# Fifteen block products for eighteen in the first product of the second mixture-of-experts layer

## The chip, the cores and the metric

The kernel runs on one core of a Trainium2 chip. The metric is the device time of one execution in microseconds, and a verdict compares medians of timed executions.

## The reference

Attention with a decaying state gives x (3072 tokens by 384), a first layer without a router turns it into a new x, and the second layer, which the change is about, mixes eight experts:

```python
logits = x @ w_gate                       # 3072 x 8
P = np.exp(logits - logits.max())
for _ in range(8):                        # alternate row and column normalisation
    P /= P.sum(1, keepdims=True) + 1e-09
    P /= P.sum(0, keepdims=True) + 1e-09
    P *= N / E
for e in range(E):                        # E = 8, w1: 384 x 1024, w2: 1024 x 384
    h = np.maximum(x @ w1[e], 0.0)
    out += P[:, e:e + 1] * (h @ w2[e])
```

## The kernel before

All matrix products of the layers are made in a split form: a float32 number is kept as a high part (`_hi`, type fp32r) and the rest (`_lo`), and a product is three matmuls, hi by hi, hi by lo and lo by hi (`split_product`, lines 843 to 846).

The program has two stretches. In the first one (lines 1011 to 1037) attention and the first layer are interleaved in slices; at its end x lies transposed in SBUF as `x2` (3 blocks of 128 features by 3072 tokens). The second layer then runs as 48 units: expert e (8) outside, 512 tokens t (6) inside. A unit has eight steps f, one for each 128 hidden features:

- TensorE, `hidden` (L1047): 3 feature blocks by 3 matmuls of 512 columns into one of the two PSUM banks of `psH`;
- ScalarE (L563): relu of that bank into `h_hi`; VectorE (L791): the rest into `h_lo`;
- TensorE, `project` (L1060), one step behind: 4 token blocks j by 3 matmuls of 384 columns. Here the tokens are the stationary operand, so that y comes out with tokens on the partitions, in the four banks of `psY`, where it stays through the unit.

After a unit VectorE multiplies each `psY` bank with that token's share `Pm` and adds it to `acc` (L821). The weights of an expert come in one DMA of 3 MB, `wx_raw`; ScalarE and VectorE split them for the next expert between their other work (`split_weights`). The normalisation of P (`over_rows`, `over_columns`, eight times) lies on VectorE in the first two units, one iteration a step, with one small matmul each time (`add_columns`, L1044). GpSimd does four casts and the maximum over partitions (L397) and nothing after. The output goes out by four DMAs of 192 KB at the end (L338), the rest before.

The order on each engine is the order of the code; between engines there are only semaphores. Units after the opening are hardware loops (`Fori`).

## Time and profile before

| | us |
|---|---|
| median of 3 runs (2159.74 to 2161.33) | 2160.88 |
| the profiled execution's own time | 2158.51 |
| its span, first to last instruction | 2156.7 |
| TensorE (PE) busy | 2129.9 |
| VectorE (DVE) busy | 772.6 |
| ScalarE (ACT) busy | 572.2 |
| GpSimd (POOL) busy | 83.3 |

The granted TensorE clock is 1.000 over the whole span. A matmul's duration in a row contains its way through the array, so consecutive matmuls overlap; their pace is the distance between the starts. The same holds, less strongly, for the other engines.

### The profile page before, as it was taken

What the parts mean: (1) busy time and instruction counts of PE and PEld (TensorE: products, weight loads), DVE (VectorE), ACT (ScalarE), POOL (GpSimd) and SP (SyncE); (2) the same over time, 40 slices, a digit from 0 to 9 for tenths busy, and PEclk for the clock granted to TensorE, in tenths of its full rate; (3) what the DMA queues carried; (4) which work ended last, traced back from release to release, by engine and by line L of the source; (5) the groups of instructions that cost most, each with busy time, mean ns of one, the idle gap of its engine ahead of it and who ended that gap; (6) DMA issues with size and microseconds to landing.
All of it is one profiled execution on the core that took longest, in us unless ns stands there. A gap on an engine that the chain in (4) does not pass through costs nothing.

```text
span 2156.7 us, 41592 instructions
## 1 busy us (share of the span) xinstructions
PE 2129.9 (99%) x17692; PEld 1934.5 (90%) x17692; DVE 772.6 (36%) x1321; ACT 572.2 (27%) x1032; POOL 83.3 (4%) x99
## 2 busy tenths in 40 slices
PE   7899999999999999999999999999999999999999
PEld 4699999999899999999999999999999999999998
DVE  3666666663632322232223222222322232223222
ACT  4555556553311211121112112111211121112111
POOL 2111121111000000000000000000000000000000
PEclk9999999999999999999999999999999999999999
DMA  8411212101100010010001000100000010000000
GB/s 201 82 43 33 56 43 51 47 5 62 60 1 0 0 59 0 0 58 0 0 0 58 0 0 0 58 0 0 29 30 0 0 58 0 0 0 15 15 29 29
DMA packets 28919, 60.53 MB, mean 28 GB/s; under 512 B 3728, under 2 KB 26000, under 8 KB 27792
## 3 DMA queue, kind: packets, MB, share of 16 engines
q1 hardware_dynamic: 28128, 58.52, 9.4%
q8 instruction: 83, 1.36, 0.3%
q10 hardware_dynamic: 688, 0.48, 0.1%
q14 instruction: 20, 0.16, 0.0%
HBM read 53.09 MB, written 4.72 MB: 27 GB/s over the span
## 4 chain that ended last, share of the span: by engine, by line
PE 98%; DMA 1%; DVE 0%; issue 0%; SPq 0%; ACT 0%; DVEq 0%
PE ps L844 30%; PE ps L846 30%; PE ps L845 30%; PE ps L917 2%; PE ps L867 2%; PE ps L956 1%; PE ps L958 1%; DMA w_raw<-moe_w 1%; PE ps L939 1%; PE ps L928 0%; PE ps L879 0%; PE ps L911 0%; PE ps L856 0%; DMA R<-rT 0%; PE ps L1001 0%
## 5 line engine op out<-in xcount | busy, mean ns | idle before, releaser
L791 DVE SCALAR_TENSOR_TENSOR h_lo<-ps,h_hi 128x512 fp32r<-128x512 f32 x384 | 265.7, 692 | 1076.9 <-ACT h_hi L563 1076.5
L563 ACT ACTIVATE h_hi<-ps 128x512 fp32r<-128x512 f32 x384 | 230.3, 600 | 1317.8 <-PE ps L846 1317.8
L846 PE MATMUL ps<-wx_hi,h_lo 128*128 128x384 f32 x1536 | 517.6, 337 | 0.0
L844 PE MATMUL ps<-wx_hi,h_hi 128*128 128x384 f32 x1536 | 516.9, 337 | 0.0
L845 PE MATMUL ps<-wx_lo,h_hi 128*128 128x384 f32 x1536 | 515.5, 336 | 0.0
L846 PE MATMUL ps<-x_hi,wx_lo 128*128 (+1 forms) x1152 | 454.9, 395 | 0.0
L845 PE MATMUL ps<-x_lo,wx_hi 128*128 (+1 forms) x1152 | 454.1, 394 | 0.0
L844 PE MATMUL ps<-x_hi,wx_hi 128*128 (+1 forms) x1152 | 448.6, 389 | 0.0
L844 PEld LDWEIGHTS ps<-wx_hi,h_hi 128*128 128x128 f32 x1536 | 288.6, 188 | 14.9 <-issue 0.2
L845 PEld LDWEIGHTS ps<-wx_lo,h_hi 128*128 128x128 f32 x1536 | 288.3, 188 | 14.4
L846 PEld LDWEIGHTS ps<-wx_hi,h_lo 128*128 128x128 f32 x1536 | 288.1, 188 | 0.0
L846 PEld LDWEIGHTS ps<-x_hi,wx_lo 128*128 128x128 f32 x1152 | 216.0, 188 | 46.1
L845 PEld LDWEIGHTS ps<-x_lo,wx_hi 128*128 128x128 f32 x1152 | 216.1, 188 | 37.6
L844 PEld LDWEIGHTS ps<-x_hi,wx_hi 128*128 128x128 f32 x1152 | 216.5, 188 | 35.8
L844 PE MATMUL ps<-x_hi,wab_hi 128*128 128x256 f32 x576 | 171.7, 298 | 0.0
L846 PE MATMUL ps<-x_hi,wab_lo 128*128 128x256 f32 x576 | 162.9, 283 | 0.0
L845 PE MATMUL ps<-x_lo,wab_hi 128*128 128x256 f32 x576 | 162.8, 283 | 0.0
L402 ACT ACTIVATE Rpad<-R 64x512 f32<-64x512 f32 (+1 forms) x170 | 110.5, 650 | 142.8 <-DVE R L640 135.7
L844 PEld LDWEIGHTS ps<-x_hi,wab_hi 128*128 128x128 f32 x576 | 109.8, 191 | 4.7 <-issue 1.9
L821 DVE SCALAR_TENSOR_TENSOR acc<-ps,Pm,acc 128x384 f32 (+1 forms) x168 | 92.8, 611 | 55.9 <-PE ps L846 55.6
L845 PEld LDWEIGHTS ps<-x_lo,wab_hi 128*128 128x128 f32 x576 | 109.9, 191 | 0.1
L846 PEld LDWEIGHTS ps<-x_hi,wab_lo 128*128 128x128 f32 x576 | 109.8, 191 | 0.0
(100 smaller groups left out, 1589.1 us busy)
## 6 DMA issues: line engine op xcount, KB each, us to landing
wx_raw<-w SPq DMA_DIRECT2D x8, 3072.0 KB, 10.2
K<-kT SPq DMA_DIRECT2D x24, 192.0 KB, 3.8
R<-rT SPq DMA_DIRECT2D x24, 192.0 KB, 4.5
V<-v_rows SPq DMA_DIRECT2D x12, 384.0 KB, 3.2
Wt<-wT SPq DMA_DIRECT2D x22, 192.0 KB, 3.9
w_raw<-moe_w SPq DMA_DIRECT2D x8, 512.0 KB, 11.3
out<-acc SPq DMA_DIRECT2D x5, 768.0 KB, 3.5
wab_raw<-moe_w SPq DMA_DIRECT2D x4, 576.0 KB, 11.7
```

Source lines behind the costliest of these rows:

```text
L402: return nc.scalar.activation(dst, src, ACT.Copy)
L563: nc.scalar.activation(h_hi[:, f % RING, :], psH(f), ACT.Relu).then_inc(h_hi_made, 1)
L791: ve.scalar_tensor_tensor(out=h_lo[:, f % RING, :], in0=psH(f), scalar=0.0, in1=h_hi[:, f % RING, :].bitcast(f32), op0=ALU.max, op1=ALU.su ...
L821: ve.scalar_tensor_tensor(out=rows, in0=psY(j), scalar=share, in1=rows, op0=ALU.mult, op1=ALU.add).then_inc(y_added, 1)
L844: mm(o, w_hi, x_hi, start=start, stop=False, skip_group_check=shared)
L845: mm(o, w_hi, x_lo, start=False, stop=False, skip_group_check=shared)
L846: return mm(o, w_lo, x_hi, start=False, stop=stop, skip_group_check=shared)
L867: last = mm(ps[:, W_bank(f), 0:D], w3T[m // HB % TURNED][:, j % HB, :], wout_raw[:, j, :], start=(j == 0), stop=(j == NF - 1))
L917: last = mm(o, keys, r, start=True, stop=True)
L939: last = mm(ps[rows:rows + HROW, tail_bank(c), HD * g:HD * g + HD], Ktok[:, c, P * g + rows:P * g + rows + HROW], V[u % 2][:, c, head:head ...
L956: last = mm(o[h], V[u % 2][:, c, head:head + HD], AT[:, 2 * (NCH * g + c) + h, :], start=True, stop=(before is None))
L958: last = mm(o[h], before[:, g, :], Rpad[u % 2][:, g, h, CH * c:CH * c + CH], start=False, stop=True)
```

## The change

**The products.** For a group of three hidden blocks f and 1024 tokens (two halves of 512), the before kernel makes 3 x 3 x 2 = 18 block products of 128 x 128 weights with 128 x 512 tokens. The new one makes 15, `S1, R1, S2, R2, S3, R3, S4, R4, S5, Q1, S6, Q0, S7, Q5, S8`, numbered 0 to 14 in the order in which TensorE makes them. Each multiplies a sum of weight blocks with a sum of x blocks. The sums of x (`xs_hi`, `xs_lo`, 15 tiles of 512 tokens) are made once for each stretch of 1024 tokens, three times in all; the sums of weights (8 of 128 columns, and 7 single blocks) for each group. The 64 blocks f of the eight experts (NF2) are run as one series: one block alone by six products (`multiply_first`), then 21 groups. So there are 3 stretches of 22 groups G, 63 of them full.

**The banks.** Only two PSUM banks serve the products: even numbers S (bank 0), odd numbers R (bank 1). Some products start a bank anew and others add to what stands in it. Product p waits until p - 2 has been taken out of its bank; S1 follows S8 in the same bank. Six products are copied out by ScalarE (`COPIED`), nine are added to or subtracted from tiles `tb` in SBUF by VectorE (`ADDED`). From the ninth product on each step finishes one of the six hidden tiles b (`LAST_ADDED`); ScalarE then makes `h_hi` and VectorE, one step later, `h_lo`, now both from SBUF.

**The second product** is turned: w2 is stationary and 512 tokens of h are moving, y comes out transposed in six banks, one for each half T and feature block d, and stays there through all eight blocks f of an expert. A projection (3 matmuls) follows each product, two of them after S3, Q1 and S8, 14 projections behind at the start of a group. When an expert ends, VectorE multiplies each of the six banks with `Pb`, P spread over the partitions, into a ring `tmp` of four (`take_y`), and GpSimd adds that to `acc`, which takes the place of x2 (`add_y`). Since eight is no multiple of three, the six `take_y` fall in three places: at R4 to Q0 of a group (6 experts), at S7 to R1 of the next (9), at S2 to S4 (8), and at the very end (1).

**GpSimd** now makes the sums of x and of weights and all low parts of the w1 operands, adds y, and has the maximum over partitions between. P goes through DRAM once and comes back broadcast, 512 KB for each expert and stretch. The rows of `acc` are turned back on TensorE: 48 transposes of 128 columns beside the next stretches, 24 at the end. The loops are written out, nothing is a hardware loop. The sums of P over rows stay where TensorE needs them in bank 1, so each of the eight column sums holds an R product back until `cs_taken`.

```diff
-    RING = 2
-    PU = NF - 1 + NJ
+    NF2 = E * NF
+    NG = 1 + (NF2 - 1) // 3
+    SINKHORN = 8
+    S1, R1, S2, R2, S3, R3, S4, R4, S5, Q1, S6, Q0, S7, Q5, S8 = range(15)
+    X_OWN = {S1: 1, R3: 2, S5: 5}
+    X_SUM = {R1: (0, 1), R2: (2, 1), R4: (2, 3), Q1: (1, 3), S6: (5, 2), Q0: (0, 2), S7: (4, 5), Q5: (3, 5), S8: (2, 4)}
+    X_LESS = (R2, S6)
+    ADDED = {S3: 1, R4: 2, S5: 4, Q1: 0, S6: 2, Q0: 1, S7: 3, Q5: 4, S8: 5}
+    LAST_ADDED = {Q1: 0, S6: 2, Q0: 1, S7: 3, Q5: 4, S8: 5}
+    FINISHED = [0, 2, 1, 3, 4, 5]
+    W2_RING, TMP = 4, 4
...
+            upto = lambda q: q + 1 + (q >= S3) + (q >= Q1)
+            if G % NG == 0:
+                return max(0, 3 * block_no(G) - upto(Q0) + p + 1)
+            return max(0, 3 * block_no(G) - upto(Q0) + upto(p) + (p == S8))
+        COLUMNS_AT = [(1, S6), (1, S8), (2, S1), (2, S6), (2, S8), (3, S1), (3, S6), (3, S8)]
...
+            def add_y(n):
+                T, d = y_tile(n)
+                pool.wait_ge(y_taken, n + 1)
+                if n // 6 % E == 0:
+                    pool.wait_ge(p_loaded, 16 * (n // 6 + 1))
+                    gp.tensor_tensor(y_acc(n), y_acc(n), Pb[:, T, :], ALU.mult).then_inc(y_added, 1)
+                else:
+                    pool.wait_ge(y_added, n - 5)
+                    plus(y_acc(n), y_acc(n), tmp[:, tmp_no(n) % TMP, :]).then_inc(y_added, 1)
+                    continue
+                if G > 1:
+                    sum_late(G)
+                    split_late(G)
+                ys = [n for p in range(NP) for n in ys_after((G, p))]
+                soon = [n for n in ys if y_at[n][1] <= S3 and n >= 6]
+                for n in soon:
+                    add_y(n)
+                if g == NG - 1 and st + 1 < NST:
+                    sum_first(st + 1)
+                    sum_xw(st + 1)
+                    for p in x_summed_in(st + 1):
+                        sum_x(st + 1, p)
+                    split_first(st + 1)
+                if full_no(G) + 1 < (NG - 1) * NST:
+                    after = full_at(full_no(G) + 1)
+                    sum_early(after)
+                    split_early(after)
+                for n in ys:
+                    if n >= 6 and n not in soon:
+                        add_y(n)
...
-                    u = e * NT + t
-                    act.wait_ge(hidden_made, u * NF + f + 1)
-                    if not (opening and f < RING):
-                        act.wait_ge(proj_done, proj_after(u, f - RING) if f >= RING else proj_after(u - 1, f - RING + NF))
-                    nc.scalar.activation(h_hi[:, f % RING, :], psH(f), ACT.Relu).then_inc(h_hi_made, 1)
...
+
+            def take_h(G, p):
+                b = LAST_ADDED[p]
+                act.wait_ge(added, add_no(G, p))
+                free_slot(G, b)
+                nc.scalar.activation(h_hi[:, b, :], tb[:, t_of(G, b), :], ACT.Relu).then_inc(h_hi_made, 1)
+                for p in range(NP):
+                    if p in COPIED:
+                        copy_product(G, p)
+                    if p in LAST_ADDED:
+                        take_h(G, p)
+                    if p == R2 and G > 1:
+                        take_late(G)
+                    if G == 1 and p == R2:
+                        route()
+                    if (G, p) == P_TURN:
+                        act.wait_ge(p_turned_made, 1)
+                        copy(p_turned[0:NTT // 2 * E, :, :], ps[0:NTT // 2 * E, 1, 0:2 * P].rearrange("p (h t) -> p h t", t=P)).then_inc(p_copied, 1)
+                    if p == S4:
+                        take_w2(G)
+                    if p == S6 and g + 1 < NG:
+                        take_early(full_at(full_no(G) + 1))
+                    if g == NG - 1 and st + 1 < NST:
+                        if p == S3:
+                            take_first(st + 1)
+                        if p >= 2:
+                            take_xs(st + 1, p - 2)
...
-                for f in range(NF):
-                    dve.wait_ge(h_hi_made, u * NF + f + 1)
-                    ve.scalar_tensor_tensor(out=h_lo[:, f % RING, :], in0=psH(f), scalar=0.0, in1=h_hi[:, f % RING, :].bitcast(f32),
-                                            op0=ALU.max, op1=ALU.subtract).then_inc(h_split, 1)
-                        ve.scalar_tensor_tensor(out=rows, in0=psY(j), scalar=share, in1=rows, op0=ALU.mult, op1=ALU.add).then_inc(y_added, 1)
...
+            def add_product(G, p):
+                b = ADDED[p]
+                t, bank = tb[:, t_of(G, b), :], bank_of(p)
+                dve.wait_ge(multiplied, product_no(G, p))
+                if p in (S3, R4, S7, S8):
+                    ve.tensor_tensor(t, t, bank, ALU.subtract).then_inc(added, 1)
+            def split_h(G, b, what):
+                dve.wait_ge(h_hi_made, h_no(G, b))
+                ve.scalar_tensor_tensor(out=h_lo[:, b, :], in0=what, scalar=0.0, in1=h_hi[:, b, :].bitcast(f32),
+                                        op0=ALU.max, op1=ALU.subtract).then_inc(h_split, 1)
+            def take_y(n):
+                T, d = y_tile(n)
+                dve.wait_ge(projected, last_projection(n) + 1)
+                    dve.wait_ge(p_loaded, 16 * (n // 6 + 1))
+                    if m >= TMP:
+                        dve.wait_ge(y_added, y_of_tmp(m - TMP) + 1)
+                    ve.tensor_tensor(tmp[:, m % TMP, :], ps[:, y_bank(T, d), :], Pb[:, T, :], ALU.mult).then_inc(y_taken, 1)
...
+                for p in range(NP if g else NL1):
+                    if step_before.get((G, p)) in COLUMNS_AT:
+                        over_columns(it)
+                    if g and p in ADDED:
+                        add_product(G, p)
+                    if split_now is not None:
+                        split_h(G, split_now, tb[:, t_of(G, split_now), :])
+                        split_now = None
+                    if g and p in LAST_ADDED:
+                        split_now = LAST_ADDED[p]
+                    for n in ys_after(step_before.get((G, p))) if (G, p) in step_before else ():
+                        take_y(n)
+                    if g and p == Q1:
+                        split_w2(G)
+                    if g == NG - 1 and st + 1 < NST and p >= 3:
+                        split_xs(st + 1, p - 3)
...
-                for k in range(KD):
-                    cols = slice(P * k, P * k + P)
-                    last = split_product(psH(f), wx_hi[:, f, cols], wx_lo[:, f, cols], high[:, k, :], x2_lo[:, k, x], k == 0, k == KD - 1)
-                last.then_inc(hidden_made, 1)
-                    last = split_product(psY(j), h_hi[:, f % RING, toks], h_lo[:, f % RING, toks],
-                                         wx_hi[:, f, D:2 * D], wx_lo[:, f, D:2 * D], f == 0, f == NF - 1)
...
+                if p >= S2:
+                    if p - 2 in COPIED:
+                        pe.wait_ge(copied, copy_no(G, p - 2))
+                    else:
+                        pe.wait_ge(added, add_no(G, p - 2))
+                elif G % NG == 1:
+                    pe.wait_ge(h_split, h_no(G - 1, p))
+                else:
+                    pe.wait_ge(added, add_no(G - 1, S8 if p == S1 else Q5))
+                triple(bank_of(p), w_hi, w_lo, xs_hi[:, p, :], xs_lo[:, p, :], p in (S1, R1, Q1, Q0, Q5), True).then_inc(multiplied, 1)
...
+                if d == 0:
+                    pe.wait_ge(w2_split, m + 1)
+                    pe.wait_ge(h_split, h_no(G, b))
+                if f % NF == 0:
+                    y = 6 * (E * (G // NG) + f // NF - 1) + 3 * (1 - T) + d
+                    if y >= 0:
+                        pe.wait_ge(y_taken, y + 1)
...
+                for p in range(NP):
+                    multiply(G, p)
+                    if (G, p) in COLUMNS_AT:
+                        add_columns(COLUMNS_AT.index((G, p)))
+                    if (G, p) == P_TURN:
+                        turn_p()
+                    project_to(projections(G, p))
+                if G in PUT_AT:
+                    done_st, j = PUT_AT[G]
+                    pe.wait_ge(y_added, 6 * E * (done_st + 1))
+                    pe.wait_ge(added, add_no(G, Q5))
+                    turn_rows(j, 1)
...
```

On TensorE, in the middle of a unit, the last matmuls of `hidden` and the first of `project` before:

```order
L846 MATMUL ps<-x_hi,wx_lo 128x512
L844 MATMUL ps<-x_hi,wx_hi 128x512
L845 MATMUL ps<-x_lo,wx_hi 128x512
L846 MATMUL ps<-x_hi,wx_lo 128x512
L1062 REGISTER_ALU
L844 MATMUL ps<-wx_hi,h_hi 128x384
L845 MATMUL ps<-wx_lo,h_hi 128x384
L846 MATMUL ps<-wx_hi,h_lo 128x384
L844 MATMUL ps<-wx_hi,h_hi 128x384
L845 MATMUL ps<-wx_lo,h_hi 128x384
```

and in a full group now, where L1438 to L1440 are the three matmuls of `triple` (`xs` a product, `h` a projection, `own` and `sum` the weight operands of w1, `w_hi` here the tile of w2):

```order
L1440 MATMUL ps<-xs_hi,sum_lo 128x512
L1438 MATMUL ps<-h_hi,w_hi 128x512
L1439 MATMUL ps<-h_lo,w_hi 128x512
L1440 MATMUL ps<-h_hi,w_lo 128x512
L1438 MATMUL ps<-xs_hi,own_hi 128x512
L1439 MATMUL ps<-xs_lo,own_hi 128x512
L1440 MATMUL ps<-xs_hi,own_lo 128x512
L1438 MATMUL ps<-h_hi,w_hi 128x512
L1439 MATMUL ps<-h_lo,w_hi 128x512
L1440 MATMUL ps<-h_hi,w_lo 128x512
L1438 MATMUL ps<-xs_hi,own_hi 128x512
L1439 MATMUL ps<-xs_lo,own_hi 128x512
```

Nine and twelve matmuls between changes of work have become three and three, all of 512 columns, and each product begins with a wait for a bank.

On VectorE, in the first unit of an expert before (L607 are the low parts of the next weights, L791 `split_h`, L821 the four additions of y):

```order
L791 SCALAR_TENSOR_TENSOR h_lo<-ps,h_hi 128x512
L607 TENSOR_TENSOR wx_lo<-wx_raw,wx_hi 128x768
L791 SCALAR_TENSOR_TENSOR h_lo<-ps,h_hi 128x512
L607 TENSOR_TENSOR wx_lo<-wx_raw,wx_hi 128x768
L791 SCALAR_TENSOR_TENSOR h_lo<-ps,h_hi 128x512 x6
L821 SCALAR_TENSOR_TENSOR acc<-ps,Pm,acc 128x384 x4
```

and in group 6 now, from product S5 to S7, where an expert ends (L1173 and L1169 `add_product`, L1177 `split_h`, L996 the low parts of w2, L1190 `take_y`):

```order
L1171 TENSOR_TENSOR tb<-ps,tb 128x512
L1190 TENSOR_TENSOR tmp<-ps,Pb 128x512
L1173 TENSOR_TENSOR tb<-ps,tb 128x512
L1190 TENSOR_TENSOR tmp<-ps,Pb 128x512
L996 TENSOR_TENSOR w_lo<-w_raw,w_hi 128x384 x3
L1173 TENSOR_TENSOR tb<-ps,tb 128x512
L1177 SCALAR_TENSOR_TENSOR h_lo<-tb,h_hi 128x512
L1190 TENSOR_TENSOR tmp<-ps,Pb 128x512 x2
L1173 TENSOR_TENSOR tb<-ps,tb 128x512
L1177 SCALAR_TENSOR_TENSOR h_lo<-tb,h_hi 128x512
L1190 TENSOR_TENSOR tmp<-ps,Pb 128x512
L1169 TENSOR_TENSOR tb<-tb,ps 128x512
```

The six `take_y`, which stood together after a unit, now stand between the additions that free the product banks; the fifth and sixth wait for GpSimd's first and second `add_y`, because `tmp` has four places.

On GpSimd, at the start of the second layer before:

```order
L389 MEMSET wg 128x96
L390 MEMSET ones 128x128
L393 CAST wx_hi<-wx_raw 128x768
L395 CAST x_hi<-x_49 128x1536
L393 CAST wx_hi<-wx_raw 128x768
L395 CAST x_hi<-x_49 128x1536
L397 ISA
L397 ISA allmax<-rowmax 128x1
```

and now, in the last group of the first stretch (G = 21): `split_late`, then the sums for the next 1024 tokens (`first_sum`, `xw`, `xs_sum`):

```order
L578 TENSOR_TENSOR own_lo<-w_raw_125,own_hi 128x128
L578 TENSOR_TENSOR own_lo<-w_raw_125,own_hi 128x2x128
L578 TENSOR_TENSOR sum_lo<-w_sum,sum_hi 128x512
L578 TENSOR_TENSOR first_sum<-first_raw 128x128 x2
L578 TENSOR_TENSOR first_sum<-first_sum,first_raw 128x128
L581 TENSOR_TENSOR xw<-x_49 128x512
L581 TENSOR_TENSOR xw<-xw,x_49 128x512
L581 TENSOR_TENSOR xs_sum<-x_49 128x512
L581 TENSOR_TENSOR xs_sum<-xw,x_49 128x512
L578 TENSOR_TENSOR xs_sum<-x_49 128x512
```

GpSimd was empty from there on; now 38 instructions and more stand in such a group. ScalarE in the same group (L834 `take_xs`, the high parts of the new x sums; L717 copies) has the first of the sums between the late weights and the copy of product R3:

```order
L717 ACTIVATE own_hi<-w_raw_125 128x128
L717 ACTIVATE own_hi<-w_raw_125 128x2x128
L717 ACTIVATE sum_hi<-w_sum 128x512
L834 ACTIVATE xs_hi<-xs_sum 128x512
L717 ACTIVATE first_hi<-first_raw 128x384
L717 ACTIVATE first_hi<-first_sum 128x256
L834 ACTIVATE xs_hi<-xs_sum 128x512
L717 ACTIVATE tb<-ps 128x512
```

The copy of R3 (the last row) stands behind the waits of `take_xs` and `take_first` for GpSimd's sums.

## Rows read from the trace of the kernel before

**Rows 1.** The page: the chain that ended last, by engine and by line.
```profile
PE 98%; DMA 1%; DVE 0%; issue 0%; SPq 0%; ACT 0%; DVEq 0%
PE ps L844 30%; PE ps L846 30%; PE ps L845 30%; PE ps L917 2%; PE ps L867 2%; PE ps L956 1%; PE ps L958 1%; DMA w_raw<-moe_w 1%; PE ps L939 1%; PE ps L928 0%; PE ps L879 0%; PE ps L911 0%; PE ps L856 0%; DMA R<-rT 0%; PE ps L1001 0%
```
**Rows 2.** PE's waits between 480 and 640 us: total, times, longest.
```profile
PE ps L1044 <- DVE csum L773: 0.6, 1, 0.6
```
**Rows 3.** Stretches: length, then busy us (instructions) by engine; PEclk, DMA share, GB/s.
```profile
0.00:400.00 400.00, 377.05 (x7349) 338.56 (x7350) 242.82 (x466) 218.39 (x422) 68.04 (x79) 1.00 0.31 71
1000.00:1500.00 500.00, 500.00 (x2515) 453.77 (x2514) 131.49 (x196) 83.71 (x136) 0.00 (x0) 1.00 0.03 13
```
**Rows 4.** PE in order of time: start, duration, line; hidden and projection of one step.
```profile
621.86 0.39 PE L844 MATMUL ps<-x_hi,wx_hi 128*128 x1
...
623.71 0.39 PE L846 MATMUL ps<-x_hi,wx_lo 128*128 x1
623.94 0.33 PE L844 MATMUL ps<-wx_hi,h_hi 128*128 128x384 f32 x1
...
626.04 0.39 PE L844 MATMUL ps<-x_hi,wx_hi 128*128 x1
```
**Rows 5.** Groups by line: count | busy, mean ns | idle before, releaser.
```profile
L791 DVE SCALAR_TENSOR_TENSOR h_lo<-ps,h_hi 128x512 fp32r<-128x512 f32 x384 | 265.7, 692 | 1076.9 <-ACT h_hi L563 1076.5
L563 ACT ACTIVATE h_hi<-ps 128x512 fp32r<-128x512 f32 x384 | 230.3, 600 | 1317.8 <-PE ps L846 1317.8
L607 DVE TENSOR_TENSOR x_lo<-x,x_hi 128x512 fp32r<-128x512 f32 x3 | 2.0, 685 | 0.0
L393 POOL CAST wx_hi<-wx_raw 128x768 fp32r<-128x768 f32 x2 | 1.7, 828 | 8.0 <-DMA wx_raw<-w 8.0
L395 POOL CAST x_hi<-x 128x1536 fp32r<-128x1536 f32 x2 | 3.1, 1568 | 0.0
```
**Rows 6.** ACT, POOL and DVE in order of time, around 563, 162 and 195 us.
```profile
562.80 0.60 ACT L563 ACTIVATE h_hi<-ps 128x512 fp32r<-128x512 f32 x1 [2.31 <-PE ps L846]
563.29 0.84 ACT L402 ACTIVATE wx_hi<-wx_raw 128x768 fp32r<-128x768 f32 x1
...
162.29 1.26 POOL L376 CAST x_hi<-xT 128x768 fp32r<-128x768 f32 x1 [4.36 <-DMA xT<-yT]
...
162.17 0.69 DVE L640 TENSOR_TENSOR R<-R,decay 128x512 f32<-128x512 f32 x1
162.77 1.32 DVE L642 TENSOR_TENSOR K<-K,decay 128x512 f32<-128x512 f32 x1
...
194.08 2.13 POOL L359 COPY Rpad<-R 64x1024 f32<-64x1024 f32 x2 [26.11 <-PE ps L958]
...
195.24 1.25 DVE L607 TENSOR_TENSOR ab_lo<-ab,ab_hi 128x256 fp32r<-128x256 f32 x1 [3.21 <-ACT ab_hi L402]
```
**Rows 7.** Opening of the second layer: PE, DVE, POOL, ACT in order of time.
```profile
543.67 0.40 PE L844 MATMUL ps<-x_hi,wx_hi 128*128 128x512 f32 x1
...
552.29 0.36 DVE L799 TENSOR_REDUCE rowmax<-ps 128x1 f32<-128x192 f32 x1 [0.39 <-PE ps L1008]
...
552.75 0.36 POOL L397 PARTITION_ALL_REDUCE allmax<-rowmax  x1 [33.14 <-DVE rowmax L799]
...
559.11 0.19 ACT L566 ACTIVATE negmax<-allmax 128x1 f32<-128x1 f32 x1
```
**Rows 8.** DVE in order of time: one normalisation of P.
```profile
569.21 0.17 DVE L778 TENSOR_SCALAR cden<-ps 128x8 f32<-128x8 f32 x1
...
571.37 0.55 DVE L773 TENSOR_REDUCE csum<-Pm 128x8 f32<-128x192 f32 x1
```
**Rows 9.** PE in order of time: four transposes of 128 columns.
```profile
26.50 0.66 PE L856 MATMUL ps<-const_sb,w_raw 128*128 128x128 f32 x4 [0.29 <-DMA w_raw<-moe_w]
```
**Rows 10.** The end: last matmul, and the last output DMAs with median time to landing.
```profile
2153.08 0.34 PE L846 MATMUL ps<-wx_hi,h_lo 128*128 128x384 f32 x1
...
2152.78 1.92 SPq L338 DMA_DIRECT2D out<-acc  x4
```

796 lines of the change are left out of this document (547 added, 249 removed).

## The prediction, made before the changed kernel was run

> **What bounds the kernel now.** I read the chain that ended last first [rows 1]: 98% of it is TensorE, and its three long lines are the split matmuls. The list of PE's waits comes next [rows 2]: in 160 us around the start of the second layer there is one wait, 0.6 us, and from 640 us on the list is empty. The stretches say the same: 500.00 us of 500 busy with 2515 matmuls, VectorE and ScalarE at 131 and 84 us, GpSimd at nothing [rows 3]. So the second layer is a pure stream of matmuls, and its time is their number times their pace. The clock is granted at its upper level, 2.4 GHz, throughout.
>
> The pace is the distance between starts [rows 4]. Nine matmuls of 512 columns take 623.94 - 621.86 = 2.08 us, 0.2311 us each; the twelve of 384 columns after them take 626.04 - 623.94 = 2.10 us, 0.175 each. A unit has 72 and 96 of them: 16.6 + 16.8 = 33.4 us, and 500 us / 2515 x 168 gives 33.4 too. 48 units are 1603 us.
>
> **What the change removes on TensorE.** Products: 3 x (6 + 21 x 15) = 963 triples. Projections: 3 x 64 x 6 = 1152 triples. Together 6345 matmuls of 512 columns, at 0.2311 us 1466 us. That is 137 us less, 121 of it from the 567 products saved, the rest since the projections go in fewer, longer matmuls. The pace of a 512-column form is in the trace, so the bound of this term is only 3 us either way. That a wait comes every three matmuls instead of nine I cost at nothing while it is fulfilled: the last product before a change, which carries the semaphore, is followed after 0.23 us like every other [rows 4].
> The Trainium skill, TensorE: Matmul & The Clock Gate, "The cost: per-tile semaphore tail", gives 26 ns for each increment. By that rule, with 2115 increments for about 912, the sum would be 32 us higher; the row shows no such gap, and it is a rival below.
>
> The written-out program costs nothing either: in the first 400 us, also written out, PE fetched and ran 7349 matmuls [rows 3], three times as dense as the second layer will be.
>
> **The other engines' prices.** A 512-wide VectorE operation takes 0.69 us to its end from PSUM and 0.685 from SBUF [rows 5], and the next starts 0.60 later (162.17 and 162.77 in [rows 6]); ScalarE 0.60, next after 0.50 [rows 5, 6]. From a product's last start to a reader's result I count 0.3 + 0.69 us. No GpSimd operation with two tensor inputs is in the trace. Nearest are the casts, one input: 0.83 us for 768, 1.57 for 1536 [rows 5], so 0.14 + 0.9 ns a column, 0.6 us for 512. Below it can't be; three times that, 1.8, is my upper bound. It has to read twice as much, so I take twice the column price: 1.1 us for 512, 0.83 for 384, 0.37 for 128. The Trainium skill, GPSIMD Engine Reference, "Elementwise — side-by-side cycle accounting", has 4497 ns for 2048 columns of such an add, which is an estimate of 1.1 us for 512 and would leave the sum as it is.
>
> The second price is a conflict: a VectorE operation with two SBUF inputs waits for a running GpSimd one. `ab_lo`, 256 wide, took 1.25 us beside a GpSimd copy, longer than the 0.69 of twice the width, and of two 512-wide products the one beside a GpSimd cast took 1.32 us instead of 0.69, and that cast 1.26 for 768 columns instead of 0.83 [rows 5, 6]. Before, `h_lo` was read from PSUM; now it has two SBUF inputs, six times a group.
>
> **A full group, replayed.** A step is a product and a projection, 6 x 0.2311 = 1.39 us, three steps have 2.08: 22.9 us. Count from the end of Q1. VectorE adds Q1 at 0.3, splits w2 until 2.3, adds S6 2.37, splits 2.97, adds Q0 3.76, splits 4.36 to 5.05. ScalarE is done with the next early weights at 4.8, and GpSimd's `split_early` wants 0.83 + 0.37 + 1.1 us: its first runs 5.05 to 5.88 behind that split. VectorE's next split waits until 5.88, the add of Q5 ends 7.13, the last split meets the 512-wide GpSimd one (6.9 to 8.0), and S8, ready at 7.9, is added by 9.3. S1 could start 2 projections after S8, at 9.02: **0.3 us lost a group, 19 us for 63**. If GpSimd comes a little later the order turns and nothing is lost; bounds 5 and 60. ScalarE (12 x 0.5 and some 5 us of weights) and GpSimd (about 11 us of 22.9) have room.
>
> **Ends of experts.** In the 6 groups where an expert ends at R4 to Q0, VectorE's fifth `take_y` needs GpSimd's first `add_y`, which stands behind `split_early` (done at about 8.0): 9.1. The adds of S6 and Q0 are through, but the add of S7, for which product S8 waits, stands behind that `take_y`: S8 starts 3.6 us late. The next splits run against GpSimd's adds of 1.1 and cost 1.9 more at S1: 5.5 x 6 = 33. Nine experts end at S7 to R1: one `take_y` before the add of S8, 0.8 x 9 = 7. Eight at S2 to S4, where VectorE has gaps: 2. **42 us**, bounds 15 and 85.
>
> **Opening.** GpSimd has 13 operations of 512 columns and 25 smaller ones, about 30 us, before the first group. It begins with the last eight slices, 8 x 27 matmuls of 256 columns at about 0.12 us or 26 us, and the first block adds 543.67 [rows 7] + 6 x 0.69 + 1.9 for what lies between = 549.7: just in time. In the first group the steps have no projections up to R4, 0.69 us against 0.95 for a copy: 1 us. The maximum over partitions took no longer than 559.11 - 552.65 = 6.5 us to reach ScalarE before [rows 7], and nobody waited; now ScalarE's copy of R3 is behind it, and product R4 could start at 555.6: I take 4, bounds 1 and 8. The normalisation is 2.7 us of VectorE (569.21 to 571.92 in [rows 8]): R product Q0 waits for `cs_taken` and the adds behind it are late, 2 us x 3; at S1 of groups 2 and 3 the second column sum comes only one step after the first, 3.3 x 2; turning P, 2. **19 us**, bounds 10 and 30.
>
> **The two changes of stretch.** ScalarE's copy of R3 stands behind the first x sum; GpSimd gets there after its late weights, at about 9.5 us before the end of Q1 plus 2 x 2.2 + 1.1 + 2 x 1.1 + 1.1: 5 us late. Then 10 more sums of 1.1 us and 15 VectorE splits share one port, and the first product of the new stretch waits for `split_first` behind the last sum: 6 more. **11 x 2 = 22 us**, bounds 10 and 45.
>
> **Small ones.** Transposes: (0.66 - 0.27) / 3 = 0.13 us each [rows 9], 48 are 6 us, with waits 8 (5 to 14). The tail before was 2156.7 - 2153.3, about 3.4 us, one VectorE operation and a 192 KB DMA of 1.92 us [rows 10]. Now come three more GpSimd adds that lag behind PE's pace (1.1 against 0.69), transposes and copies: **+5** (3 to 9).
>
> **The sum**, made against the profiled execution's 2158.5 (its span is 2156.7): -137 + 19 + 42 + 19 + 22 + 8 + 5 = -22, 2136.5. The median shown is 2.4 us above that execution, so I expect 2139.
>
> **The rivals.**
> 1. The forecast, stalls of 90 to 135 us: 2110 to 2156. Chance 0.41.
> 2. The work beside PE stays hidden. For it: the averages leave room everywhere (VectorE about 13 us of 22.9), the conflicts depend on who comes first, and a late stream opens slack for the next group. Against it: the in-order queue in front of S8's add has no slack in steps S6 to S8. All terms at their low bounds: 5 + 15 + 10 + 10 + 5 + 3 = 48 of 137, 2160.9 - 89 = 2072; I put this case at 2070 to 2110. Chance 0.28.
> 3. GpSimd becomes the bound: slower. If a 512-wide GpSimd operation takes 1.8 us, `split_early` needs 3.9 us instead of 2.3, is done 1.6 us later than above, just after S1's nominal start, and each VectorE split beside it waits up to 1.8: about 1.7 us lost a group instead of 0.3, +88, and the adds at expert ends, the sums between stretches grow by 0.7 x (6 x 4 + 2 x 12) = 34: 2139 + 122 = 2261. It decides from 0.3 + (22 + 4) / 63 = 0.7 us a group on. Against it: the casts' own 0.9 ns a column. Chance 0.21.
> 4. The increments show (the page's rule above): some 1200 x 26 ns, 2139 + 32 = 2171. The starts in [rows 4] speak against it. Chance 0.03.
> 5. The change doesn't do what it says, because the products' pace falls back: a matmul that waits for its bank restarts the array, say 0.3 us at each of 963 products, 289 us; [rows 2, 4] show changes of bank without a gap, so I leave it within the 0.21.
> Between 2156.5 and 2165 lies what a measurement of this kernel can't tell from no change (0.2% of 2160.9 is 4.3 us): chance 0.07.
>
> **Range.** Faster 0.41 + 0.28 = 0.69, same 0.07, slower 0.21 + 0.03 = 0.24. For 8 in 10 I leave 0.07 below 2080 and 0.13 above 2193, inside rivals 2 and 3. The forecast's own range is 2110 to 2156.
>
> **What the profile after would show.** PE's matmuls (17692 of the whole kernel before) fewer by 48 x 168 - 6345 = 1719, plus 74 transposes; 0.231 us between starts within a group; PE busy near 2000 us, and about 100 us in waits, which it hardly had: for VectorE's `tb` (L1169) at S1, the longest group; in the six groups named, waits of 2 to 4 us at S8 and a VectorE idle in front of L1190 released by POOL; some 5 us for ScalarE's `tb` in groups 21 and 43. GpSimd about 750 us busy, with 1.1 us a 512-wide `x2`. Wrong would make me: a pace other than 0.231; `h_lo` from SBUF at 0.69 without the 1.2 us ones (rival 2); GpSimd operations of 0.6 us (rival 2) or 1.8 (rival 3); waits of PE for `w1_split` rather than for `tb`.

## The result, and the profile after

The change made the kernel 1.5% slower. Median of 4 executions 2192.76 us (2190.82 to 2194.69) against 2160.31 (2159.73 to 2161.33): ratio 1.015, interval 1.0132 to 1.0167. I had put 2139 and a range of 2080 to 2193, with 0.24 for slower. That 2192.8 still lies in that range, by 0.2 us, is luck: the forecast was a gain, and its own range ended at 2156. One of the four executions of the run on the changes of stretch below fell into a slow state of the chip (3301.67 us at a granted clock of 0.557) and is left out of its numbers.

The page of after: busy times, then the chain that ended last, by engine and by line.

```profile
PE 2048.4 (93%) x16047; PEld 1688.8 (77%) x16047; DVE 1298.6 (59%) x2007; ACT 999.4 (46%) x1982; POOL 1160.8 (53%) x1553
...
PE 59%; POOL 16%; issue 12%; DVE 9%; ACT 2%; DMA 1%; POOLq 0%; ACTq 0%; DVEq 0%; SPq 0%
```

The chain was 98% TensorE before [rows 1]. Now a quarter of it is GpSimd and VectorE. The same stretch as in [rows 3]:

```profile
1000.00:1500.00 500.00, 464.99 (x1965) 370.75 (x1964) 293.30 (x405) 217.88 (x431) 329.10 (x448) 0.98 0.22 58
```

TensorE is idle for 35 of 500 us, GpSimd went from nothing to 329 us, and the clock is no longer granted in full (0.98). PE's waits in the second layer (540 us to the end), which were a single one of 0.6 us in [rows 2]: total, times, longest.

```profile
PE ps L1438 <- DVE tb L1169: 72.0, 61, 3.6
PE ps L1438 <- ACT tb L717: 15.2, 4, 6.4
PE ps L1438 <- POOL first_lo L578: 6.7, 3, 3.1
PE ps L1513 <- DVE csum L1142: 6.3, 2, 3.3
```

The account of the second layer, from the starts of its matmuls: 6345 of them, the first at 544.23, the last at 2180.7 (before: 543.67 and 2153.08). Their distance is 0.231 us (median), so 1465.7 us of the 1636.5 is the stream; 171 us is lost. Some 20 us of that is not waiting but matmuls at half the pace (below). The tail behind the last matmul is 10.2 us instead of 3.6. So 544.2 + 1465.7 + 171 + 10.2 makes the span of 2190.9.

Where the 171 us are: group lengths, from the first matmul of S1 to the next group's. A plain group (one without an expert's end, behind the opening and away from the changes of stretch) has 99 matmuls, a stream of 22.87 us.

| groups (count) | us each | lost, us | predicted |
|---|---|---|---|
| what a plain group loses, counted for groups 6 to 64 but for the four of the last line (55) | 23.25 | 21 | 19 |
| end of an expert at R4 to Q0 (6), and the groups behind | 30.4, then 23.2 or 24.6 | 47 more | 33 |
| end at S7 to R1 (8, the ninth is in the opening), and the groups behind | 23.8, then 25.5 | 22 more | 7 |
| end at S2 to S4 (8) | 25.0 | 14 more | 2 |
| groups 0 to 5, the opening | 6.2, 23.4, 32.9, 32.2, 25.1, 25.7 | 32 | 19 |
| groups 21, 22 and 43, 44, the changes of stretch | 38.3 and 10.4 | 35 | 22 |

Group 6, where the first of the six ends lies: GpSimd, VectorE and TensorE in order of time (start, duration).

```profile
709.15 1.88 POOL L578 TENSOR_TENSOR own_lo<-w_raw,own_hi 128x384 fp32r<-128x384 f32 x2 [6.24 <-ACT sum_hi L717]
...
709.58 1.12 DVE L1177 SCALAR_TENSOR_TENSOR h_lo<-tb,h_hi 128x512 fp32r<-128x512 f32 x1
...
710.99 1.26 POOL L578 TENSOR_TENSOR sum_lo<-w_sum,sum_hi 128x512 fp32r<-128x512 f32 x1
712.21 8.33 POOL L581 TENSOR_TENSOR x<-x,tmp 128x512 f32<-128x512 f32 x6
713.60 0.69 DVE L1190 TENSOR_TENSOR tmp<-ps,Pb 128x512 f32<-128x512 f32 x1 [2.90 <-POOL x L581]
714.21 0.68 DVE L1169 TENSOR_TENSOR tb<-tb,ps 128x512 f32<-128x512 f32 x1
714.80 1.69 DVE L1177 SCALAR_TENSOR_TENSOR h_lo<-tb,h_hi 128x512 fp32r<-128x512 f32 x1
...
714.94 0.50 PE L1438 MATMUL ps<-xs_hi,sum_hi 128*128 128x512 f32 x1 [3.56 <-DVE tb L1169]
```

One reads it from the bottom up. Product S8 waits 3.56 us for the add of S7 (L1169). That add could have run at 711, but in VectorE's queue the fifth `take_y` (L1190) is ahead of it. `take_y` waits 2.90 us for the first of GpSimd's six adds, which starts only at 712.21, behind `split_early` (709.15 to 712.25). The `h_lo` that follow take 1.69 us beside the adds instead of 0.69.

What happens to TensorE's clock there (length, then busy us and instructions of PE, PEld, DVE, ACT, POOL; granted clock, DMA share, GB/s):

```profile
707.00:711.00 4.00, 3.72 (x17) 2.73 (x15) 3.71 (x6) 2.40 (x5) 1.85 (x3) 1.00 0.54 154
711.00:714.70 3.70, 0.38 (x2) 0.00 (x0) 1.10 (x2) 0.00 (x0) 3.70 (x5) 1.00 0.00 0
716.30:719.70 3.40, 1.92 (x5) 0.83 (x3) 3.40 (x5) 0.63 (x1) 3.40 (x3) 0.50 0.15 39
```

TensorE stood from 711.4 to 714.9, and from 716.3 on the clock is granted at 0.50, its lower level of 1.2 GHz, when TensorE has work again. There are 14 such stretches from the opening on, 66.9 us, each behind TensorE's idle times or at the end: in groups 2 and 3, behind all six ends at R4 to Q0, at both changes of stretch. Some 100 matmuls in them started about 0.43 us apart instead of 0.231: about 10 us behind the six ends, 7 at the changes of stretch, 4 in the opening. Before, the clock was 1.00 throughout.

The prices (count | busy, mean ns | idle before):

```profile
L1177 DVE SCALAR_TENSOR_TENSOR h_lo<-tb,h_hi 128x512 fp32r<-128x512 f32 x378 | 370.3, 983 | 11.5 <-ACT h_hi L930 11.0
L581 POOL TENSOR_TENSOR x<-x,tmp 128x512 f32<-128x512 f32 x126 | 173.4, 1405 | 35.5 <-DVE tmp L1190 35.5
L578 POOL TENSOR_TENSOR sum_lo<-w_sum,sum_hi 128x512 fp32r<-128x512 f32 x126 | 162.2, 1287 | 0.0
...
L1190 DVE TENSOR_TENSOR tmp<-ps,Pb 128x512 f32<-128x512 f32 x126 | 82.7, 682 | 60.6 <-PE ps L1440 30.4 <-POOL x L581 30.2
```

Alone, GpSimd takes 1.26 to 1.31 us for 512 columns with two inputs (priced 1.1), and `h_lo` 0.98 in the mean instead of the 0.69 of [rows 5]. `tmp`, which is read from PSUM, stays at 0.68.

### The profile page after: what moved, and what is told of

Same layout as the page of the kernel before. It is cut to its first block, busy times and chain, and to the rows that moved or that the text cites. A ratio compares the mean times of both kernels' runs of the same rounds, so it can differ in the third digit from the quotient of the medians.

```text
span 2190.9 us, 41117 instructions
## 1 busy us (share of the span) xinstructions
PE 2048.4 (93%) x16047; PEld 1688.8 (77%) x16047; DVE 1298.6 (59%) x2007; ACT 999.4 (46%) x1982; POOL 1160.8 (53%) x1553
## 4 chain that ended last, share of the span: by engine, by line
PE 59%; POOL 16%; issue 12%; DVE 9%; ACT 2%; DMA 1%; POOLq 0%; ACTq 0%; DVEq 0%; SPq 0%
PE ps L1438 13%; PE ps L1440 12%; PE ps L1439 12%; PE ps L1242 5%; PE ps L1243 4%; PE ps L1244 4%; DVE h_lo L1177 4%; POOL w_sum L578 4%; POOL x L581 3%; POOL own_lo L578 3%; PE ps L1315 2%; POOL sum_lo L578 2%; PE ps L1265 2%; DVE tb L1169 2%; POOL w_sum L581 1%
## 5 line engine op out<-in xcount | busy, mean ns | idle before, releaser
L930 ACT ACTIVATE h_hi<-tb 128x512 fp32r<-128x512 f32 x378 | 236.4, 629 | 523.6 <-DVE tb L1173 373.8
L1438 PE MATMUL ps<-h_hi,w_hi 128*128 128x512 f32 x1152 | 460.0, 399 | 0.2 <-DVE h_lo L1177 0.2
L1440 PE MATMUL ps<-h_hi,w_lo 128*128 128x512 f32 x1152 | 459.8, 399 | 0.0
L1439 PE MATMUL ps<-h_lo,w_hi 128*128 128x512 f32 x1152 | 456.2, 396 | 0.0
L1169 DVE TENSOR_TENSOR tb<-tb,ps 128x512 f32<-128x512 f32 x252 | 172.1, 683 | 465.5 <-PE ps L1440 461.8
L1177 DVE SCALAR_TENSOR_TENSOR h_lo<-tb,h_hi 128x512 fp32r<-128x512 f32 x378 | 370.3, 983 | 11.5 <-ACT h_hi L930 11.0
L717 ACT ACTIVATE tb<-ps 128x512 f32<-128x512 f32 x378 | 225.1, 598 | 322.7 <-PE ps L1440 315.8
L1438 PE MATMUL ps<-xs_hi,sum_hi 128*128 128x512 f32 x504 | 207.1, 411 | 77.1 <-DVE tb L1169 72.0
L1439 PEld LDWEIGHTS ps<-h_lo,w_hi 128*128 128x128 f32 x1152 | 222.4, 193 | 49.9
L1438 PEld LDWEIGHTS ps<-h_hi,w_hi 128*128 128x128 f32 x1152 | 219.3, 190 | 52.8 <-issue 4.4
L1440 PEld LDWEIGHTS ps<-h_hi,w_lo 128*128 128x128 f32 x1152 | 219.4, 190 | 48.7
L1440 PE MATMUL ps<-xs_hi,sum_lo 128*128 128x512 f32 x504 | 201.5, 400 | 0.0
L1173 DVE TENSOR_TENSOR tb<-ps,tb 128x512 f32<-128x512 f32 x252 | 173.3, 688 | 43.9 <-PE ps L1440 40.1
L1438 PE MATMUL ps<-xs_hi,own_hi 128*128 128x512 f32 x441 | 176.9, 401 | 20.3 <-ACT tb L717 15.2
L1438 PEld LDWEIGHTS ps<-xs_hi,sum_hi 128*128 128x128 f32 x504 | 95.2, 189 | 126.6 <-issue 69.4
L1440 PE MATMUL ps<-xs_hi,own_lo 128*128 128x512 f32 x441 | 175.6, 398 | 0.0
L717 ACT ACTIVATE Rpad<-R 64x512 f32<-64x512 f32 (+1 forms) x170 | 110.5, 650 | 142.7 <-DVE R L1029 135.2
```

The lines of the kernel that those rows point to most:

```text
L717: return nc.scalar.activation(dst, src, ACT.Copy)
L930: nc.scalar.activation(h_hi[:, b, :], tb[:, t_of(G, b), :], ACT.Relu).then_inc(h_hi_made, 1)
L1169: ve.tensor_tensor(t, t, bank, ALU.subtract).then_inc(added, 1)
L1173: ve.tensor_tensor(t, bank, t, ALU.add).then_inc(added, 1)
L1177: ve.scalar_tensor_tensor(out=h_lo[:, b, :], in0=what, scalar=0.0, in1=h_hi[:, b, :].bitcast(f32), op0=ALU.max, op1=ALU.subtract).then_inc ...
L1438: mm(o, w_hi, x_hi, start=start, stop=False, skip_group_check=True)
```

## The experiments

Two theories. **Queues** (theory 1 in the expectations): what stands ahead of what on GpSimd and VectorE makes the waits, and the clock falls behind them. **Port** (theory 2): GpSimd's operations with two inputs and VectorE's from SBUF keep each other waiting, so that the work costs the same wherever it stands. All runs change only the second layer. A number of microseconds "less" is against the 2192.76 of the kernel after. The group lengths of all of them are in one table behind the last run.

### Two adds earlier

```diff
                     sum_early(after)
+                    for n in ys:
+                        if n >= 6 and y_at[n][1] in (R4, S5):
+                            soon.append(n)
+                            add_y(n)
                     split_early(after)
```

> Only GpSimd's order changes: in the six groups in which an expert ends at R4 to Q0, its first two adds of y stand ahead of split_early (where GpSimd is idle for 6 us) instead of behind it. Theory 1 (the queue in front of the add that S8 waits for is the cause of these groups' 30.4 us, and the clock's fall to 1.2 GHz follows from the idle TensorE): the wait of 3.7 us at S8 is gone, the S1 behind it is late by less than 1 us, the six stretches at the lower clock behind these groups are gone; a group takes 24 to 25 us, and the time falls by 28 to 38 us, to about 2160. Rival (the cost is GpSimd's own price and the shared port, and the work only lands elsewhere): the wait moves to S7, Q5 or the next S1 and the time falls by less than 10 us.

2171.32 us (2167.65 to 2175.29), 21 less. The six groups take 26.6 instead of 30.4 us; their waits of 3.7 at S8 are 0.7 now, and none of the clock's falls behind these groups is left. But S7 and Q5 now wait 0.5 and 0.9 us (0 and 0.4 in after): `w_lo` and `h_lo` meet the adds. TensorE's longest wait for `add_product` is 1.8 instead of 3.6 us:

```profile
PE ps L1442 <- DVE tb L1173: 49.8, 60, 1.8
```

So the queue theory holds for the long wait and for the clock, and 21 of the 28 to 38 us that I expected come; the new waits take the rest. (In the total of stretches at the lower clock the six are made up for by others, 62.0 us; two of them lie in the first layer, at 21 and 66 us, and come and go between executions.)

### All adds placed between the weights' work

```diff
+            PLACES = {R4: "ccdAAA", S7: "dAAAcc", S2: "abcccd"}
...
                     sum_late(G)
+                    adds(G, "a")
                     split_late(G)
+                adds(G, "b")
...
                     sum_early(after)
+                    adds(G, "c")
                     split_early(after)
+                adds(G, "d")
```

Capital letters, and the last two of S7, mean the next group; `tmp` has five buffers.

> All adds of y are given places between GpSimd's four weight steps, by the step at which the expert ends, with at most one behind split_early, and tmp gets a fifth buffer. Theory 1: groups with an expert's end cost 0.5 to 1 us over a plain one, so of about 50 + 22 + 14 us lost there 60 to 70 are won, with the clock: 2192.8 - 65 = about 2128, between 2120 and 2140. Rival: the adds beside VectorE's splits cost the same wherever they stand: 2155 or more.

2171.36 us (2169.66 to 2173.24): no more than the two adds alone, and the rival (2155 or more) was right, not the forecast of 2128. The groups behind S7 ends gain 0.8 us, those with S2 ends lose 1.1 (S7 waits 1.75 us where adds run beside VectorE's splits). Moved along GpSimd's queue, the adds met other operations of VectorE.

### GpSimd light

```diff
-                less(own_lo[:, 1:4, :], raw[:, 2:5, :], own_hi[:, 1:4, :].bitcast(f32))
+                gp.memset(own_lo[:, 1:4, :].bitcast(f32), 0.0)
...
-                    plus(y_acc(n), y_acc(n), tmp[:, tmp_no(n) % TMP, :]).then_inc(y_added, 1)
+                    plus(y_acc(n)[:, 0:16], y_acc(n)[:, 0:16], tmp[:, tmp_no(n) % TMP, 0:16]).then_inc(y_added, 1)
```

> GpSimd's low parts of the first product's weights become fills with zero (no input), and its adds and products for y take 16 of 512 columns; order and waits stay. Leaves out: the low parts of these weights and most of the sum over experts. Theory 2 (GpSimd's two-input operations, by their length and by holding up VectorE's splits with two SBUF inputs, make most of the lost time): h_lo takes 0.69 us beside them, the 0.4 us lost at S1 of a plain group goes, S8's wait falls under 0.5 us, and the time falls by 80 to 110 us, to 2085 to 2110; what stays is the opening and the two changes of stretch, whose sums are not touched. Rival (the order of the queues alone costs it, whatever the operations take): S8's wait stays above 2 us and the time falls by less than 40 us.

2088.22 us (2084.66 to 2089.72), 105 less, within the 80 to 110 forecast. The kernel leaves out the low parts of these weights and most of the sum over the experts. Order and semaphores are those of after, yet S8 waits 0.6 us in the six groups, plain groups lose nothing, and no fall of the clock follows them. So it is the length of GpSimd's operations, by the queue and by the port, and not the order by itself. The six groups still take 25.1 us, 2.2 more than plain ones. Three rows show length and port (the first is a wait: total, times, longest):

```profile
PE ps L1438 <- DVE tb L1169: 9.4, 17, 0.8
...
L1177 DVE SCALAR_TENSOR_TENSOR h_lo<-tb,h_hi 128x512 fp32r<-128x512 f32 x378 | 280.9, 752 | 0.2
...
L639 POOL MEMSET sum_lo<- 128x512 f32 x63 | 33.2, 527 | 0.0
```

The opening (26.8 a group) and the changes of stretch (36.7) mostly stayed, as expected.

### VectorE's splits with one input

```diff
-                ve.scalar_tensor_tensor(out=h_lo[:, b, :], in0=what, scalar=0.0, in1=h_hi[:, b, :].bitcast(f32),
-                                        op0=ALU.max, op1=ALU.subtract).then_inc(h_split, 1)
+                ve.tensor_scalar(h_lo[:, b, :], what, 0.0, 0.001, ALU.max, ALU.mult).then_inc(h_split, 1)
```

and `w2_lo` likewise. Neither is the real low part any more, but a scaled copy.

> VectorE's h_lo and w2_lo become operations with one input (max and a small factor), so that the part below the high one is not computed but a scaled copy; GpSimd is untouched at its two inputs. Theory 2a (VectorE and GpSimd wait for each other only where both read two SBUF inputs): VectorE's splits take under 0.7 us throughout, GpSimd's 512-wide adds stay near 1.27 us without the ones of 1.7, plain groups lose under 0.1 us at S1; the wait at S8 in six groups stays (it is GpSimd's queue), shorter by about 0.5 us; the time falls by 25 to 45 us, to 2150 to 2168. Rival 2b (any VectorE operation from SBUF conflicts): the splits still show 1.1 to 1.8 us and the time falls by less than 10 us.

2129.08 us (2127.09 to 2130.85), 64 less: more than either theory. VectorE in group 6 of this run, in order of time:

```profile
699.75 0.42 DVE L1177 TENSOR_SCALAR h_lo<-tb 128x512 fp32r<-128x512 f32 x1
...
701.88 1.14 DVE L1177 TENSOR_SCALAR h_lo<-tb 128x512 fp32r<-128x512 f32 x1
...
707.12 1.42 DVE L1177 TENSOR_SCALAR h_lo<-tb 128x512 fp32r<-128x512 f32 x1
```

Theory 2a has fallen: these operations have one input and still take 1.14 and 1.42 us beside GpSimd. Alone they take 0.42, not 0.69 as with two inputs; with 378 of them I take that for what was won, together with shorter holds for GpSimd's adds (1.45 beside them instead of 1.71). No run separates the two. The S8 wait stayed at 3.5 us, as the queue theory has it, and with it the clock's fall in five of the six groups.

The Trainium skill, SBUF — State Buffer, "SBUF: two separate sides", says that VectorE and GpSimd share a pair of ports as an exclusive lock held for a whole instruction, taken by a VectorE operation with two SBUF inputs or in a two-port mode; VectorE: DVE Perf Modes, "Mode 2×_2P — use both read ports for one tensor", says that this mode is one tensor read through both ports. The rows agree: 0.42 us for a lone one-input split, 1.14 and 1.42 beside GpSimd. I had used the first half of that rule and forgotten the second.

### The adds of y on VectorE, the rest as it was

```diff
+            ADDS = {S7: [(1, R1), (1, R1), (1, S2), (1, S2), (1, R2), (1, R2)],
+                    R4: [(0, S5), (1, R1), (1, R1), (1, S2), (1, S2), (1, R2)],
+                    S2: [(0, R2), (0, S3), (0, R3), (1, R1), (1, R1), (1, S2)]}
...
+                    for n in adds_at.get((G, p), ()):
+                        add_y(n)
```

This stands in VectorE's loop, with an `add_y` of its own; (1, R1) is step R1 of the next group. `tmp` has five buffers.

> The changed kernel with one thing undone in part: the adds of y (126 of 512 columns, all but those of the first and the last expert) are VectorE's again, one behind the first product of y, the others in the gaps that VectorE has at R1 to R2 and R3; tmp has five buffers. GpSimd keeps the sums and low parts of weights. Theory (GpSimd's adds, 1.27 us each in a queue with the weights and on the shared port, are what the ends of experts cost): the groups with R4 ends take 24.5 instead of 30.4 us, those behind S7 ends 23.4 instead of 25.5, S2 ends 23.5 instead of 25, plain groups stay at 23.25: about 75 us less, 2118, between 2105 and 2135. Rival (VectorE has no room for 12 operations of 0.6 us in such a group): 2160 or more.

2135.36 us (2133.99 to 2136.51), 57 less and now under the kernel before: 0.989 (0.9875 to 0.9906). The forecast was 2118, between 2105 and 2135. The groups behind S7 ends take 23.3 us and those with S2 ends 23.2: nothing of theirs is left. R4 ends are 26.3 instead of my 24.5: Q5 waits 0.9 us and S8 0.7 there with no add on GpSimd. VectorE's own queue is fuller there than I thought (GpSimd light left 25.1 us), but two `h_lo` of group 6 still met GpSimd's low parts (1.12 and 0.99 us), and the run doesn't separate the two. The list of waits, with the first row of after at 27 instead of 72 us:

```profile
PE ps L1452 <- DVE tb L1162: 26.9, 57, 1.7
PE ps L1452 <- ACT tb L710: 15.1, 4, 6.4
```

### The weights' low parts on VectorE

```diff
-                    if g and p == Q1:
+                    if g and p == R4:
                         split_w2(G)
+                    if g and p == R3 and G > 1:
+                        split_late(G)
+                    if p == Q1 and 0 < g < NG - 1:
+                        split_early(full_at(full_no(G) + 1))
```

in VectorE's loop, and GpSimd's calls gone; ScalarE takes the early weights at S5 instead of S6.

> The low parts of the first product's weights are made by VectorE (behind R3 and behind Q1 of a group, where it has room) and no longer by GpSimd, ScalarE takes the early weights at S5 instead of S6, w2 is split behind R4; GpSimd keeps the sums of weights and the adds of y, which now follow each y at once. The same work, moved away from S7 to S1 where VectorE's own splits have no slack. Theory 2 (port conflict and GpSimd's price at that place): plain groups 22.9 instead of 23.25 us, the six groups with an end at R4 to Q0 at most 26 instead of 30.4, the others 23.5; about 2192.8 - 22 - 35 - 20 = 2115, between 2105 and 2135. Rival: VectorE, with 3.3 us more a group, becomes what TensorE waits for: 2180 or more.

2147.83 us (2146.14 to 2153.98), 45 less, not the 78 of the forecast (2115, between 2105 and 2135). Plain groups are 22.9, as expected: the 0.4 us of each was `split_early` beside `h_lo`. The six are at 26.3. Two things I had not counted. S2 ends got worse, 26.5, since four adds ahead of `sum_early` now hold back the low parts in VectorE's queue; and in group 1 VectorE's wait for the weights of group 2 stands ahead of the normalisation, 7.0 us at Q0.

```profile
PE ps L1458 <- DVE sum_lo L994: 13.0, 16, 2.1
PE ps L1458 <- DVE cden L1145: 8.2, 3, 7.0
```

### The changes of stretch

```diff
                     sum_late(G)
+                    if g == NG - 1 and st + 1 < NST:
+                        for p in (R1, S2, R2):
+                            sum_x(st + 1, p)
                     split_late(G)
...
-                    sum_first(st + 1)
-                    sum_xw(st + 1)
-                    for p in x_summed_in(st + 1):
+                    for p in (S4, R4, Q1, S6, Q0, S7, Q5):
                         sum_x(st + 1, p)
-                    split_first(st + 1)
```

`sum_first`, `sum_xw` and `split_first` stand behind groups 10 and 12 of a stretch, the sum for S8 behind `sum_early`, and ScalarE takes S8's x behind the first h.

> At the two changes of stretch only: the sums of the first block and xw are made by group 10 and 12, the sums of x follow each product's end (three of them ahead of split_late, S8's behind sum_early), and ScalarE takes S8's x behind the first h. If the order of GpSimd's queue makes the 6.5 us wait at R4 and the 3.2 us one for first_lo, both go; the 15 VectorE splits beside 11 sums of 1.29 us stay. 38.3 us of groups 21 and 43 become about 29, 10.4 of groups 22 and 44 about 9: 20 to 25 us less, about 2170. Rival (the shared port is what costs there): the waits move to S7, Q5, S8, and less than 8 us are won.

2180.11 us (median of three, 2180.09 to 2189.28), 13 less: between the forecast (20 to 25 less) and the rival (under 8). It is still slower than the kernel before (interval of the ratio 1.0091 to 1.0146). In the trace, groups 21 and 43 went from 38.3 to 30.1 us and 22 and 44 from 10.4 to 8.9, 19 us together; the 6.4 us for ScalarE's `tb` and the 3.1 for `first_lo` are gone, S7 waits 2.7 instead of 1.7. The mechanism is the one named. The median shows 13 of the 19 us; in the profiled execution the second layer began 2.6 us later than in that of after, and groups 1 to 4 and one plain group took 5 us more. That spread between executions is the limit of what I can say of the rest. What after looked like there:

```profile
1076.29 1.26 POOL L581 TENSOR_TENSOR xs_sum<-x 128x512 f32<-128x512 f32 x1
...
1077.64 0.63 ACT L834 ACTIVATE xs_hi<-xs_sum 128x512 fp32r<-128x512 f32 x1 [7.84 <-POOL xs_sum L581]
...
1079.42 0.57 ACT L717 ACTIVATE tb<-ps 128x512 f32<-128x512 f32 x1
...
1080.05 0.79 PE L1438 MATMUL ps<-xs_hi,own_hi 128*128 128x512 f32 x1 [6.36 <-ACT tb L717]
```

The last row is R4 waiting for the copy of R3 above it, which stood behind a high part that waited 7.84 us for GpSimd's first sum of x.

### The opening

```diff
-        COLUMNS_AT = [(1, S6), (1, S8), (2, S1), (2, S6), (2, S8), (3, S1), (3, S6), (3, S8)]
-        P_TURN = (4, S1)
+        COLUMNS_AT = [(1, S6), (2, S2), (2, S4), (2, S6), (3, S2), (3, S4), (4, S2), (4, S4)]
+        P_TURN = (4, S6)
```

Sums at S2 and S4 write into the bank in which R1 to R4 are still adding up, so this run spoils R's products; its time stands.

> Only the places of the eight column sums change: one at S6 of groups 1 and 2, the others at S2 and S4 of groups 2 to 4 where VectorE is idle, none at S1 or S8; P is turned at S6 of group 4. If the opening's 28 us (groups 1 to 4 take 113.6 us instead of 86) come from the normalisation standing in VectorE's queue in front of the adds at S8, S1 and Q0, they shrink by 12 to 20 us and the two falls of the clock in groups 2 and 3 go: about 2177 us. Rival: the 2.7 us of VectorE's work cost the same wherever they stand, or GpSimd's conflict makes the opening's loss: within 4 us of 2193.

2189.16 us, within 4 us of after, as the rival said. Groups 1 to 4 did get 11 us shorter (102.7 in sum), but group 5 took 32.0 instead of 25.7: the six products of y with P stood ahead of its weights on GpSimd, and ScalarE's copy behind those. A second attempt has the sums at S5 to S8, where R's bank is free:

```diff
+        COLUMNS_AT = [(1, S6), (1, S8), (2, S5), (2, S8), (3, S5), (3, S8), (4, S5), (4, S7)]
+        P_TURN = (5, S1)
```

> The opening once more on the changed kernel, with places at which R's bank is free: the column sums at S6 and S8 of group 1, S5 and S8 of groups 2 and 3, S5 and S7 of group 4 (so that two of them always have the 4 to 12 us between them that VectorE's 2.7 us want), P turned at S1 of group 5, and the six products of y with P between sum_early and split_early of group 5. If the opening's loss is the distance of the column sums and these six GpSimd operations in front of group 5's weights: 10 to 16 us less than 2192.8, about 2180. Rival (VectorE's 2.7 us in front of an add cost the same anywhere in a group): within 4 us of 2193.

2188.21 us (2184.80 to 2192.08). Groups 1 to 4 take 106.4 us instead of 113.6, group 5 27.3, group 6's next 25.9. So 4 or 5 us of the opening's 28 are the distance of the sums, and the largest part of its cost stays wherever the normalisation is put. The gains forecast, 12 to 20 and 10 to 16 us, were both too high, and the rivals (within 4 us of 2193) nearer: 3.6 and 4.6 us.

### Everything together

The weights' low parts on VectorE, the changes of stretch, the first opening above (with its spoilt products) and five buffers for `tmp`.

> The edits of the three runs before together, with a fifth buffer for tmp. If the three causes are separate, their gains add: 2115 - 16 - 22 = about 2078, between 2065 and 2095, so faster than the kernel before by 3 to 4%. If VectorE is the bound or the gains are one and the same stall, above 2120.

2137.90 us (2137.05 to 2139.45). 10 less than the weights' low parts alone, not 70. Then with the second opening, ScalarE and VectorE taking group 2's weights behind S8 of group 1, and adds in places of their own (three ahead of `sum_early` and three behind it for S2 ends; two behind it and four behind the next `sum_late` for the others):

> The weights' low parts on VectorE and the changed order at the changes of stretch, as in the run of all edits, and in addition the opening of the run above, the early weights of group 2 behind S8 of group 1, and places for GpSimd's adds: two behind sum_early and four behind the next sum_late where an expert ends at R4 or S7, three ahead of sum_early and three behind it where it ends at S2, so that no sum of weights is late. If the losses that stay in that run (S5 to S7 of the groups with or behind an expert's end, 7 us at Q0 of group 1, 6.5 us at R4 of group 5) are these queues: 2138 less 13 (nine groups), 24 (eight), 15 (opening) is about 2090, between 2080 and 2105. If they are the shared port, whose work only moves: above 2120.

2137.78 us (2134.63 to 2141.09): nothing from the places, again. S2 ends even grew to 27.3. This is why, in group 17 of this run:

```profile
963.66 4.09 POOL L581 TENSOR_TENSOR x<-x,tmp 128x512 f32<-128x512 f32 x3
...
965.01 2.89 DVE L1011 TENSOR_TENSOR own_lo<-w_raw,own_hi 128x384 fp32r<-128x384 f32 x2 [0.43 <-ACT sum_hi L731]
...
967.82 0.68 DVE L1011 TENSOR_TENSOR sum_lo<-w_sum,sum_hi 128x512 fp32r<-128x512 f32 x1
968.42 0.68 DVE L1204 TENSOR_TENSOR tb<-ps,tb 128x512 f32<-128x512 f32 x1
...
969.15 0.50 PE L1475 MATMUL ps<-xs_hi,own_hi 128*128 128x512 f32 x1 [2.08 <-DVE tb L1204]
```

Two low parts of 384 and 128 columns, 0.55 and 0.28 us alone, take 2.89 us beside three adds; `sum_lo`, with the adds over, takes 0.68 for 512. TensorE gets the bill behind the next add. What is left is to take the adds off GpSimd too:

> The run of all edits with the placed adds, with the adds of y on VectorE as well, so that GpSimd keeps only the sums of weights (0.46 us each), of x and what belongs to the first and last expert. In that run VectorE's w_lo, own_lo and sum_lo showed 0.8 to 1.6 us beside GpSimd's adds of 1.3. Theory 2 (every VectorE operation with two SBUF inputs waits for the running GpSimd one): groups with S2 ends 24 instead of 27.3 us, behind S7 ends 23.2 instead of 24.9, R4 ends 25 instead of 26.4: 2137.8 - 26 - 13 - 8 = about 2091, between 2080 and 2110. Rival (VectorE is full): 2130 or more.

2091.67 us (2090.82 to 2092.53), which is 101 us under after and 3.1% under the kernel before: ratio 0.9685 (0.9672 to 0.9699). The forecast was 2091, and its parts came about as forecast: S2 ends 24.0 (24), the groups behind S7 ends 23.0 (23.2), R4 ends 25.9 (25). The page of this run and the stretch of [rows 3]:

```profile
PE 2022.4 (97%) x16047; PEld 1679.4 (80%) x16047; DVE 1450.5 (69%) x2511; ACT 1009.3 (48%) x1982; POOL 657.7 (31%) x1049
```

```profile
1000.00:1500.00 500.00, 490.43 (x2113) 394.45 (x2112) 373.22 (x614) 237.53 (x462) 184.28 (x307) 1.00 0.23 62
```

VectorE does 504 operations more than in after (2511 against 2007) for 152 us more of busy time, GpSimd 504 fewer for 503 us less. The 152 are net: added up by their rows, which overlap a little, the moved operations take some 280 us there, and the 378 `h_lo`, at 0.76 instead of 0.98 us, give back 84. TensorE's idle time in this stretch falls from 35.0 to 9.6 us. The clock is granted in full there; in the whole second layer only three stretches of 1.2 GHz are left, 14.4 us, one of them at the end.

### The group lengths

Worked out from the starts of S1's first matmul (plain: medians; the others: means); the last line is what the stream alone takes. "Behind" is the group after an S7 end. In the light run plain groups without transposes take 22.74 us, 0.2297 a matmul in the mean, so the last line, from the median of 0.231, is 0.1 us a group too high.

| run | plain | R4 end | S7 end | behind | S2 end | 21, 43 | 1 to 4 | median, us |
|---|---|---|---|---|---|---|---|---|
| after | 23.3 | 30.4 | 23.8 | 25.5 | 25.0 | 38.3 | 28.4 | 2192.8 |
| two adds earlier | 23.2 | 26.6 | 23.8 | 25.5 | 24.9 | 39.3 | 28.9 | 2171.3 |
| adds placed | 23.2 | 26.7 | 23.9 | 24.7 | 26.1 | 39.0 | 28.9 | 2171.4 |
| one-input splits | 22.9 | 28.8 | 23.2 | 23.6 | 23.5 | 35.9 | 27.2 | 2129.1 |
| GpSimd light | 22.9 | 25.1 | 22.9 | 23.0 | 22.9 | 36.7 | 26.8 | 2088.2 |
| adds on VectorE | 23.3 | 26.3 | 23.8 | 23.3 | 23.2 | 38.1 | 28.9 | 2135.4 |
| low parts on VectorE | 22.9 | 26.3 | 22.9 | 24.6 | 26.5 | 33.4 | 30.3 | 2147.8 |
| changes of stretch | 23.3 | 30.4 | 23.8 | 25.5 | 25.0 | 30.1 | 29.0 | 2180.1 |
| first opening | 23.3 | 30.4 | 23.9 | 25.5 | 25.0 | 38.2 | 25.7 | 2189.2 |
| second opening | 23.2 | 30.4 | 23.9 | 25.5 | 25.0 | 38.5 | 26.6 | 2188.2 |
| all | 22.9 | 26.3 | 22.9 | 24.7 | 26.4 | 28.5 | 26.6 | 2137.9 |
| all, adds placed | 22.9 | 26.4 | 22.9 | 24.9 | 27.3 | 28.4 | 26.2 | 2137.8 |
| all, adds on VectorE | 22.9 | 25.9 | 22.9 | 23.0 | 24.0 | 28.3 | 26.2 | 2091.7 |
| the stream | 22.87 | 22.87 | 22.87 | 22.87 | 22.87 | 22.87 | 21.5 | |

## Why the prediction was wrong

**The stream was right.** 6345 matmuls at 0.231 us, within groups without a gap for the wait every three matmuls or for the increments; the term of -137 was even 6 us better, since the second layer before had taken 1609.4 us between its first and last matmul and not the 1603 of its 48 units. Rivals 4 and 5 are out. (Of the 137, the 567 saved products are 131 us, 567 x 0.2311, and not 121; the sum stands. The first layer's matmuls are four times as dense as the second's, not three.)

**The sum of what the other engines cost was too small**: 115 us predicted (19 + 42 + 19 + 22 + 8 + 5), 177 measured (171 lost between the first and the last matmul, 6.5 at the tail). Which steps failed:

1. *Ends of experts*, 42 predicted, 83 measured; the largest error, 41 of the 62 us. The wait at S8 was priced right (3.6 against 3.7, same place, same cause); of the 14 us by which the six ends came dearer (47 for 33) about 10 are matmuls at half pace behind that wait. Wrong for the others was that I stopped at the group in which the expert ends. For S7 ends I priced a `take_y` of 0.8 us; the four adds behind it stand in front of the next group's `sum_late` on GpSimd, and that group loses 2.2 us. For S2 ends I wrote that VectorE has gaps; GpSimd has none, four adds of 1.3 us stand ahead of `sum_early`, and everything behind comes late, 1.7 us a group. With the adds on VectorE both vanish (23.3 and 23.2).
2. *GpSimd's price*, 1.1 predicted, 1.26 to 1.31 alone and 1.7 beside `h_lo`; 0.46 for 128 columns instead of 0.37 and 1.02 for 384 instead of 0.83. I had twice the casts' column price (their two rows give 0.09 us and 0.96 ns a column, not 0.14 and 0.9, which leaves the 1.1 as it is); these rows give about 0.19 us and 2.15 ns a column. And GpSimd was busy 1051 us in the second layer against the 750 I wrote. The estimate of 1.1 us from the table of the Trainium skill, GPSIMD Engine Reference, "Elementwise — side-by-side cycle accounting", for 2048 columns was equally low; the trace decides.
3. *The conflict* was named, with [rows 6], but charged only where the replay of one group had two operations meet. A VectorE operation that reads SBUF alone waits out a GpSimd operation with inputs that began before it, and the other way round. That comes up everywhere: 315 of 358 `h_lo` between 640 and 2160 us met one (median 0.86 us, a tenth over 1.59), against 0.68 for the 43 that did not.
4. *The clock* was missing. I wrote that it is granted in full throughout, which was so because TensorE never stood still; my own forecast had it stand 2 to 4 us in six places and more in the opening. The falls behind these cost some 20 us. That those behind the six ends follow from the waits the runs show: with the S8 wait at 0.7 us none of the six is left, with it at 3.5 us five of six are. The Trainium skill, TensorE: Matmul & The Clock Gate, "What's actually happening", has it that throttled is the default state and activity releases it; the 0.50 behind each long wait agrees.
5. *Opening* 32 for 19 and *changes of stretch* 35 for 22: right in place and cause (3.3 us twice for `csum` at S1 and 6.4 for R4 are in the waits), too small by the clock and by GpSimd's price. *Transposes*: 8 us predicted, none visible in after, where the 16 groups with them are as long as others. In the light run, where plain groups wait for nothing, they are 23.2 us against 22.74, and all 16 together cost some 6 us, so the price was about right and is hidden in after behind waits that are there anyway. *Tail*: 5 predicted, 6.5.

**Which rival came true?** None as written. Rival 3 (GpSimd becomes the bound, slower, 0.21) has the right sign, engine and port, but its condition of 1.8 us was not met, and its 0.7 us a plain group is 0.4. The loss came from the ends of experts. The chance of 0.69 for faster was too high, as I see it, since the sum's terms all had the same unmeasured price under them, GpSimd's, and their own bounds reached further up than down (5 to 60 around 19, 15 to 85 around 42).

**What stays open.** How the 83 us of the ends divide into queue and port: the two are one chain (an operation that waits for the port makes the queue longer), and the runs move both. The opening's 25 us that are left in the best run weren't followed up, nor the 3 us that each of the R4 ends loses in it.

## What to carry to other kernels

Before work is moved to an idle engine, list for each operation behind the moved one who waits for it, into the next round too: of the 83 us at the ends of experts 22 lay in the group behind, and the prediction had nothing there for them. An engine at 53% busy is no free room when its operations hold a port that the critical engine's queue needs; here VectorE's busy time grew by 152 us for what had kept GpSimd busy for 503, and taking the work back, with the better order at the changes of stretch and in the opening, turned 1.5% slower into 3.1% faster. And a forecast that brings idle time to TensorE needs a term for the clock that falls behind it.

## What the runs showed of the hardware

- VectorE's operations with an input from PSUM don't meet GpSimd at all: `tmp` took 0.68 us (median) both in 76 cases beside a GpSimd operation and in 44 alone, and `tb` likewise (397 and 136).
- A one-input operation from SBUF of 512 columns takes 0.42 us alone, but waits for GpSimd just like one with two (a quarter of the 272 that met it over 0.99 us, up to 1.55).
- The waiting goes both ways: GpSimd's adds took 1.30 us alone (median) and 1.71 beside `h_lo`.
- GpSimd's fills with zero didn't hold VectorE up: of the `h_lo` in that run all 93 that met nothing but fills took 0.68 to 0.69 us, and the 139 that met a sum took 0.87 in the median, up to 1.2.
